# Squares folded on VectorE, a later second softmax, and expert weights loaded and split one step ahead

## The reference, cut to what matters

```python
# q, k, v: [2, 5056, 256]
qn = q / (norm(q, axis=1) + 1e-6);  kn = k / (norm(k, axis=1) + 1e-6)
s = kn.transpose(0, 2, 1) @ qn / tau            # [2, 256, 256]
a = softmax(s);  x = (v @ a).reshape(10112, 256)
# layer 1
logits = normalised(x) @ normalised(expert_emb).T / moe_tau
e = argmax(logits);  gate = softmax(logits)[e]
x = gate * (relu(x @ w1[e]) @ w2[e])
# layer 2
logits = x @ w_gate;  e = argmax(logits);  gate = softmax(logits)[e]
eom = sigmoid(x @ w_output_gate)[e]
out = gate * eom * (relu(x @ w1b[e]) @ w2b[e])
```

## Time and profile before

| | us |
|---|---|
| median of three runs | 1398.2 (1398.1 to 1405.37) |
| the profiled execution, its own time | 1400.51 |
| its span | 1398.8 |
| busy PE, DVE, ACT, POOL | 1280.1, 714.8, 497.9, 343.9 |
| share of the span on the chain that ended last: PE | 74% |
| same chain: DMA | 4% |

### The profile page before, as it was taken

One profiled execution on the slowest core, in us unless ns is written; L12 is line 12 of the kernel. 1 busy time (PEld: TensorE's weight loads), 2 busy tenths in 40 slices (PEclk: granted clock), 3 DMA queues, 4 the chain that ended last, 5 costly groups with the idle time before them and its releaser, 6 DMA issues.

```text
span 1398.8 us, 28869 instructions
## 1 busy us (share of the span) xinstructions
PE 1280.1 (92%) x10174; PEld 1249.5 (89%) x10175; DVE 714.8 (51%) x2506; ACT 497.9 (36%) x1181; POOL 343.9 (25%) x475
## 2 busy tenths in 40 slices
PE   7998853889999999999999994899999999999996
PEld 6887743879999999999999993899999999999996
DVE  5557871235555565556565562134444445444454
ACT  6448751223333233423333331233333324333333
POOL 1003773122212212221221212132222222222223
PEclk9999986999999999999999996999999999999998
DMA  8655655871111111311111115941111113111112
GB/s 314 247 196 192 216 177 187 276 263 51 46 39 39 46 33 45 99 38 33 45 41 36 46 31 189 372 128 48 45 46 46 46 42 104 42 46 46 46 50 83
DMA packets 78872, 143.88 MB, mean 103 GB/s; under 512 B 8900, under 2 KB 57679, under 8 KB 77808
## 3 DMA queue, kind: packets, MB, share of 16 engines
q1 hardware_dynamic: 54048, 92.68, 20.3%
q0 software_dynamic: 12288, 31.74, 6.1%
q10 hardware_dynamic: 12496, 18.97, 4.0%
HBM read 107.31 MB, written 38.57 MB: 104 GB/s over the span
## 4 chain that ended last, share of the span: by engine, by line
PE 74%; DMA 4%; issue 1%; SPq 1%; POOL 1%; DVE 1%; ACT 1%; DVEq 0%; POOLq 0%; ACTq 0%
PE ps L1482 32%; PE ps L1498 31%; PE ps L1391 3%; PE ps L1405 3%; PE ps L1437 2%; DMA x_in<-dispatched 2%; DMA raw<-in_moe_w_dram 2%; PE ps L1398 1%; PE ps L1428 1%; POOL dispatched L604 1%; DMA x_in_even<-dispatched 0%; SPq L374 0%; POOL w_lo L618 0%; DMA dispatched<-y_out,y_pos_i 0%; DVE w_lo L990 0%
## 5 line engine op out<-in xcount | busy, mean ns | idle before, releaser
L875 ACT ACTIVATE h_hi<-ps 128x256 fp32r<-128x256 f32 x624 | 239.6, 384 | 637.6 <-PE ps L1482 632.2
L1248 DVE SCALAR_TENSOR_TENSOR h_lo<-ps,h_hi 128x256 fp32r<-128x256 f32 x624 | 264.1, 424 | 194.7 <-ACT h_hi L875 185.7
L1498 PE MATMUL ps<-w_hi,h_hi 128*128 128x256 f32 x1248 | 362.9, 291 | 0.0
L1482 PE MATMUL ps<-xT_hi,w_hi 128*128 128x256 f32 x1248 | 360.2, 289 | 1.4 <-DVE w_lo L990 1.4
L1498 PE MATMUL ps<-w_hi,h_lo 128*128 128x256 f32 x1248 | 353.1, 283 | 0.0
L1498 PE MATMUL ps<-w_lo,h_hi 128*128 128x256 f32 x1248 | 353.1, 283 | 0.0
L1482 PE MATMUL ps<-xT_hi,w_lo 128*128 128x256 f32 x1248 | 352.8, 283 | 0.0
L1482 PE MATMUL ps<-xT_lo,w_hi 128*128 128x256 f32 x1248 | 352.7, 283 | 0.0
L1498 PEld LDWEIGHTS ps<-w_lo,h_hi 128*128 128x128 f32 x1248 | 239.0, 192 | 0.0
L1498 PEld LDWEIGHTS ps<-w_hi,h_lo 128*128 128x128 f32 x1248 | 238.8, 191 | 0.0
L1498 PEld LDWEIGHTS ps<-w_hi,h_hi 128*128 128x128 f32 x1248 | 238.7, 191 | 0.0
(11 more groups left out here) (217 smaller groups left out, 1666.7 us busy)
## 6 DMA issues: line engine op xcount, KB each, us to landing
x_in<-dispatched SPq DMA_DIRECT2D x80, 264.0 KB, 2.7
arena<-in_moe_w_dram SPq DMA_DIRECT2D x14, 1024.0 KB, 9.3
raw<-in_moe_w_dram SPq DMA_DIRECT2D x12, 1024.0 KB, 8.0
raw<-in_moe_w_dram ACTq DMA_DIRECT2D x10, 1024.0 KB, 7.4
arena<-in_q_dram SPq DMA_DIRECT2D x14, 640.0 KB, 4.9
arena<-in_k_dram SPq DMA_DIRECT2D x14, 640.0 KB, 6.3
v_sb<-in_moe_w_dram SPq DMA_DIRECT2D x8, 1024.0 KB, 7.4
v_sb<-in_v_dram SPq DMA_DIRECT2D x4, 1280.0 KB, 6.9
```

Source lines behind the costliest of these rows:

```text
L875: nc.scalar.activation(h_hi[:, c, :], h_ps(c, SUB * P), ACT.Relu).then_inc(h_hi_ready[c], 1)
L1248: V.scalar_tensor_tensor(h_lo[:, c, :], h_ps(c, SUB * P), 0.0, h_hi[:, c, :], op0=ALU.max, op1=ALU.subtract).then_inc(h_ready[c], 1)
L1482: last = T.matmul(h_ps(c, SUB * P), w1_halves[w][:, par, d, c * P:(c + 1) * P], x_halves[x][:, d, :], start=(d == 0 and at == 0), stop=(d ...
L1498: last = T.matmul(y_ps[:, s * C:(s + 1) * C], h_halves[h][:, c, s * P:(s + 1) * P], w2_halves[w][:, par, c, :], start=(c == 0 and at == 0) ...
```

## The change

Eight edits. (1) The first unit's first slot of q and of k is loaded by DMAs of its own. (2) DVE folds the five slots of `sumsq` into one by six additions, and `fold_norms` on PE shrinks from 15 products to 3. (3) The second batch's raw products are copied from PSUM to SBUF after v unit 0 (`save_s`), and `fold_norms(1)` moves from unit 0 to unit 2. (4) The rest of the second softmax moves: roots to unit 5 (beside the root of group 0), reciprocals to unit 10, scaling to 11, exponentials to 12, `make_a` to 13, the transposes and the product to units 13 to 16, and the splits to 16 and 17. The load of tail weights that waits for it moves from v group 3 to group 5. (5) SP loads only the first full expert in the prologue; ACT loads expert i + 1 before the tiles of expert i. (6) The first expert is split wholly in tail step 4 on ACT, and its w1 low half on DVE after the x of the first tile. (7) w1 and w2 of the next expert are both split behind the tiles of its predecessor, on ACT, DVE and POOL. (8) The waits for loads at a layer's end go, and two pairs of semaphores are merged.

```diff
@@ -444,6 +447,14 @@
                     sp.wait_ge(qk_squared, n - QRING + 1)
+                if n == 0:
+                    for t, src in enumerate((q[0], k[0])):
+                        rows = src[0:FULL * P, :].rearrange("(p t) c -> p t c", t=FULL)
+                        sp.dma_start(qk[:, 0, t, 0:C], rows[:, 0, :]).then_inc(qk_first, 16)
+                    for t, src in enumerate((q[0], k[0])):
+                        rows = src[0:FULL * P, :].rearrange("(p t) c -> p t c", t=FULL)
+                        sp.dma_start(qk[:, 0, t, C:].rearrange("p (t c) -> p t c", c=C), rows[:, 1:U, :]).then_inc(qk_in[0], 16)
+                    continue
                 load_unit(qk[:, n % QRING, 0, :], q[b], j, qk_in[n % QRING])
...
@@ -452,7 +463,7 @@
                     load_tail_w2(sp, 0, 0)
-                if n == 3:
+                if n == 5:
                     sp.wait_ge(a_ready, B)
...
@@ -501,14 +512,14 @@
 
-                def load_expert(r):
+                def load_first_expert():
                     sp.wait_ge(order_ready, m + 1)
...
                         sp.wait_ge(raw_free, 1)
-                    e = sp.value_load(plan[m][0:1, EXPERT, r:r + 1], min_val=0, max_val=E - 1)
-                    load_weights(sp, m, e, r)
+                    e = sp.value_load(plan[m][0:1, EXPERT, 0:1], min_val=0, max_val=E - 1)
+                    load_weights(sp, m, e, 0)
 
...
@@ -529,12 +540,11 @@
                 next_w2(5, 2)
-                load_expert(0)
+                load_first_expert()
                 next_w1(6, 3)
...
                 next_w2(7, 4)
-                load_expert(1)
 
...
@@ -655,13 +665,13 @@
 
-                def ahead(pair, par, first):
+                def behind(pair, par, first):
                     unless_last(pool, pair, par, lambda: split_w2_lo(L, pair * 2 + (par + 1), 1 - par))
...
 
-                each_tile(pool, m, nothing, body, tile, big, (ahead, None))
+                each_tile(pool, m, nothing, body, tile, big, (None, behind))
 
...
@@ -777,17 +789,17 @@
                     square_x(u - 1)
+                    if u == PAIRS:
+                        norm_roots(1)
                     if u % PAIRS == 0:
...
                     exps(u // PAIRS)
-                if u == 1:
-                    norm_roots(1)
-                if u == 4:
+                if u == 12:
                     s_exps(1)
-                if u == 8:
+                if u == 14:
                     take_aT(1)
-                if u == 10:
+                if u == 16:
                     split_a(1)
...
@@ -836,10 +845,9 @@
                             take_yT(n)
-                        if n == TP - 1:
-                            w1_piece(L, 0, 0, i)
                         if n == TP:
-                            w2_piece(L, 0, 0, i)
+                            for w in range(2):
+                                (w1_piece if i < SUB else w2_piece)(L, 0, 0, 2 * (i % SUB) + w)
                     if n < TP:
...
@@ -856,15 +864,18 @@
                     hold(act, L.w2_split_dve, 2 * pair + (par + 1))
-                    with act.If(pair < E // 2 - 1):
-                        at = nc.s_assert_le(2 * pair + (2 + par), E - 2 + par)
+
+                    def do():
+                        at = nc.s_assert_le(2 * pair + (par + 1), E - 1)
                         e = act.value_load(plan[m][0:1, EXPERT, bass.ds(at, 1)], min_val=0, max_val=E - 1)
-                        load_weights(act, m, e, par)
-                        act.reg_add(loads[par], loads[par], 1)
+                        load_weights(act, m, e, 1 - par)
+
+                    unless_last(act, pair, par, do)
 
...
                         split_w1_hi(L, pair + par, 1 - par)
+                        split_w2_hi(L, pair + par, 1 - par)
                         act.reg_add(splits, splits, 1)
...
@@ -878,13 +889,8 @@
                         y_exps(n)
-                    with act.If(t < 1):
-                        hold(act, L.tile_done, n)
-                        unless_last(act, pair, par, lambda: split_w2_hi(L, pair + par, 1 - par))
 
                 each_tile(act, m, before_expert, body, tile, big, (None, behind))
-                for r in range(2):
-                    hold(act, L.raw_in[r], act.snap(loads[r]) * 32)
                 hold(act, L.w1_split, act.snap(splits))
...
@@ -926,7 +932,11 @@
 
-            def scale_s(b):
+            def save_s(b):
+                for c in range(CC):
+                    V.tensor_copy(s_sb[:, c, :], s_ps(b, c)).then_inc(s_saved, 1)
+
+            def invert_norms(b):
                 dve.wait_ge(small_in, 80)
...
@@ -935,9 +945,12 @@
                 V.tensor_scalar(norms[:, C:], norms[:, C:], rtau[:, 0:1], None, op0=ALU.mult)
+
+            def scale_s(b):
+                dve.wait_ge(s_saved, CC * (b + 1))
                 dve.drain()
                 for c in range(CC):
-                    V.scalar_tensor_tensor(s_sb[:, c, :], s_ps(b, c), norms[:, C + c:C + c + 1], norms[:, 0:C],
+                    V.scalar_tensor_tensor(s_sb[:, c, :], s_sb[:, c, :], norms[:, C + c:C + c + 1], norms[:, 0:C],
                                                   op0=ALU.mult, op1=ALU.mult)
...
@@ -969,10 +982,20 @@
                 dve.wait_ge(square_used, b * (2 * NU - 2) + 2 * NU)
-                dve.sem_inc(sumsq_ready, 1)
+                for t in range(2):
+                    V.tensor_tensor(sumsq[:, t, 0:2 * C], sumsq[:, t, 0:2 * C], sumsq[:, t, 2 * C:4 * C], op=ALU.add).then_inc(sumsq_folded[0], 1)
+                dve.wait_ge(sumsq_folded[0], 2 * b + 2)
+                for t in range(2):
+                    V.tensor_tensor(sumsq[:, t, 0:C], sumsq[:, t, 0:C], sumsq[:, t, C:2 * C], op=ALU.add).then_inc(sumsq_folded[1], 1)
+                dve.wait_ge(sumsq_folded[1], 2 * b + 2)
+                for t in range(2):
+                    last = V.tensor_tensor(sumsq[:, t, 0:C], sumsq[:, t, 0:C], sumsq[:, t, 4 * C:], op=ALU.add)
+                last.then_inc(sumsq_ready, 1)
                 if b == 0:
...
                     V.tensor_copy(enT[:, :, :], en_ps).then_inc(enT_ready, 1)
+                    save_s(0)
+                    invert_norms(0)
                     scale_s(0)
...
@@ -1075,13 +1098,17 @@
                         split_v(ahead)
-                if u == 3:
+                if u == 1:
+                    save_s(1)
+                if u == 10:
+                    invert_norms(1)
+                if u == 11:
                     scale_s(1)
-                if u == 5:
+                if u == 13:
                     make_a(1)
-                if u == 10:
+                if u == 16:
                     take_ae(1)
-                if u == 11:
+                if u == 17:
                     split_a(1)
...
@@ -1227,16 +1254,19 @@
                         take_xT(L, n + 1)
+                        split_w1_lo(L, 0, 0)
                     if m == 0:
                         y_route_2(n)
-                    if n == TP - 1:
-                        split_w1_lo(L, 0, 0)
                     if n == TP:
...
                 def behind(pair, par, first):
-                    unless_last(dve, pair, par, lambda: split_w1_lo(L, pair * 2 + (par + 1), 1 - par))
+                    def do():
+                        split_w1_lo(L, pair * 2 + (par + 1), 1 - par)
+                        split_w2_lo(L, pair * 2 + (par + 1), 1 - par)
+
+                    unless_last(dve, pair, par, do)
                     take_y(L, dve.snap(tile))
...
@@ -1258,8 +1288,6 @@
                         y_route_2(n)
-                    with dve.If(t < 1):
-                        unless_last(dve, pair, par, lambda: split_w2_lo(L, pair * 2 + (par + 1), 1 - par))
 
...
@@ -1301,12 +1329,9 @@
                 pe.wait_ge(sumsq_ready, b + 1)
-                for t in range(U):
-                    T.matmul(norm_ps[b][0], ones[:, :], sumsq[:, 0, t * C:(t + 1) * C], start=t == 0, stop=t == U - 1)
+                T.matmul(norm_ps[b][0], ones[:, :], sumsq[:, 0, 0:C], start=True, stop=True)
                 for c in range(CC):
-                    for t in range(U):
-                        last = T.matmul(norm_ps[b][1][:, c:c + 1], sumsq[:, 1, t * C + c * P:t * C + (c + 1) * P], ones[:, 0:1],
-                                        start=t == 0, stop=t == U - 1)
+                    last = T.matmul(norm_ps[b][1][:, c:c + 1], sumsq[:, 1, c * P:(c + 1) * P], ones[:, 0:1], start=True, stop=True)
                 last.then_inc(norm_done, 1)
...
@@ -1315,8 +1340,11 @@
                         multiply_ae(0)
-                    pe.wait_ge(qk_in[j % QRING], qk_count(b, j))
                     for t in range(U):
+                        if b == 0 and j == 0 and t == 0:
+                            pe.wait_ge(qk_first, 32)
+                        elif t == (b == 0 and j == 0):
+                            pe.wait_ge(qk_in[j % QRING], qk_count(b, j))
                         r = REST if j == NU - 1 and t == U - 1 else P
...
```

(8 more changed lines are left out.)

20 lines of the change are left out of this document (11 added, 9 removed).

## The result

| | before | after |
|---|---|---|
| median | 1400.12 us (4 runs, 1398.1 to 1405.37) | 1380.47 us (4 runs, 1376.6 to 1382.84) |
| ratio | | 0.9851, 95% interval 0.9813 to 0.989 |
| the profiled execution, own time | 1400.51 | 1381.58 |
| its span | 1398.8 | 1379.8 |

The time lies in the wide range, 2.5 us inside its upper end; it is 9.5 us above the point and outside the 1364 to 1378 that the prediction gave its own sum. The profiled execution is 19 us shorter, where the sum had 27.2.

A forecast was written before the change was run, and what follows sets the result against it. PE, with 74% of the chain, bounds the kernel, so gains come only where it stands; before layer 0 the scatters bound. Terms summed to -27.2 us, 1400.5 to 1373.3, median 2.3 lower: 1371 us, 8-in-10 range 1360 to 1383.

The forecast's parts named there:

- The v stage: Ahead of layer 0: first positions 12.7 us earlier, 4.6 given back, so the stage ends 8.1 us earlier (4 to 11).
- The hole: POOL's scatters in the v stage: a gap of 4.1 us between first and second positions, before the eleventh scatter.
- The first products: Kernel start: a smaller first load lets PE do four products in advance, 0.4 us won (0.5 lost to 1.2 won).
- First fold: PE between the two batches: 6 of 30 instructions remain, 3.6 us less (3.4 to 3.8).
- Tails of layer 0 and first tile: Layer 0: waits for ACT and x go, 5.7 and 8.4 us won; the first tile's stall goes, 4.8 won.
- Changes of expert: Next expert's h_hi waits for splits: 0.3 us net won in layer 0, 3.0 lost over two changes in layer 1.
- 1.5 follows in slow products: Change of expert in layer 0: slow PE products after its stall cost 1.5 us, within 4.5 lost.
- End of layer 0: Before layer 0's last y: ACT's copy of y waits for POOL's split, 2.1 us lost (1 to 4).
- Tails of layer 1: Layer 1's tail steps: ACT's 9.92 us wait goes but DMAs are full, so 5 us won (0 to 8).
- PE waits for tail weights in step 4: Tail steps: one of the signs that would show the prediction wrong.
- changes of expert cost more: Rival, chance 0.10: POOL's pieces or ACT's hold take 2.5 us more at four places, giving 1381 us.
- The tails wait for DMA anyway: Rival, chance 0.08: weights come last in the tails, half of 19.1 us is kept, giving 1381 us.

The follow-up runs named there:

- softmax_early: The changed kernel with the second softmax back in the early units, folds on DVE and copy of raw products kept: 1379.66 us, ratio 0.9851.
- attention_part: The kernel before with edits 1 to 4 alone, expert weights loaded and split as before: 1397.56 us, ratio 0.9981.
- no_spare_split: The changed kernel without the next expert's load and splits where that expert has no full tile; engines read the tile count first: 1409.52 us, ratio 0.9817.
- dve_splits: The changed kernel with POOL's two pieces of w2's low half done by DVE at expert changes and layer ends: 1403.2 us, ratio 0.9781.
- changed_third: The changed kernel, unaltered, run again as the base in the third series: 1382.03 us, ratio 0.987 to the kernel before.
- experts_part: The kernel before with edits 5 to 8 alone, expert weights loaded and split one step ahead: 1389.77 us, ratio 0.9915.
- changed_again: The changed kernel, unaltered, run again as the base in the second series: 1381.46 us, ratio 0.9863 to the kernel before.

## Why the prediction was right, and where it was short

**The v stage** (-8.1): right in its sum in the first trace, -8.5 at the last scatter, and 1.1 and 3.5 us too much by the two others (-7.0, -4.6). The hole is where it was put and 0.5 us larger than said. What it says of causes is not all right. It booked 7.3 us as won by moving fold and softmax together, and 4.6 as given back. softmax_early shows that the softmax costs POOL's end the same at both places, so the two entries cancel but for the folds.

**The first products** (0.4 won): wrong, and outside its bounds. By the runs with the whole load the cut costs 0.9 to 2.6 us. The step that failed is "the other four slots land later by two issues": the issues are 0.95 of the 2.04 us by which they come later. Against the kernel before the fold starts 0.5 us late, against the changed kernel with the whole load 1.3. That the latter is 0.8 earlier than the kernel before, with the same load, is not explained: the same 160 products take 36.85 us in the one and 37.61 in the other.

**First fold** (-3.6): from 45.38 to the next product 0.9 us, before 4.4.

**Tails of layer 0 and first tile** (-14.1, -4.8): -14.1 and -4.7. Not foreseen was that these terms and the one of the v stage hang on each other: without them the v stage's gain was lost again in layer 0's tails, 3.9 of 4.4 us in the trace of attention_part, and the median moved by 2.2 us and not by 8.3.

**Changes of expert** (-0.3 and +3.0): the chain was right in each link, by under half a microsecond at each place: PE waits 3.48 us and not 3.0, then 1.9 and 1.7 and not 1.5. The term that was mis-sized is "1.5 follows in slow products" in layer 0 (4.8), and in layer 1, where I charged none, 1.8 each time. That makes 3.3 + 3.6 of the missing 8.2. How much it is differs from execution to execution (see the last section); that it was near its most in the profiled one is chance. Moving the guard takes waits and slow products away together.

**End of layer 0** (+2.1): +3.9. The failed step is that the last y is late through ACT's copy alone. It is late on DVE already: by DVE's own two further pieces (1.3 us), and by POOL's pieces, which hold DVE's copy of `y_id` for 2.7 us, as dve_splits shows. Leaving all splits out at this place won 5.0 us (no_spare_split), leaving out POOL's alone 0.7, as DVE took them over.

**Tails of layer 1** (-5.0): -6.0, with two waits for tail weights, 1.3 and 1.6 us, in line with the reasoning by DMA rate. The second of them is in step 4, at 884.49 us, and "PE waits for tail weights in step 4" was one of the signs of being wrong; as the term came out all the same, the sign was badly chosen for this layer.

**The rivals.** The time came out, in part by chance, at that of "changes of expert cost more" (1381, chance 0.10): 9.2 us more than forecast at those four places, where the rival had 10. Its mechanism accounts for a part: POOL and DVE hold each other up at the end of layer 0, and POOL's scatter at the change is 0.5 us long for it. The larger part is the clock, 6.9 of the 9.2 us. The Trainium skill (SBUF — State Buffer, Who interferes with whom, and SBUF: two separate sides) says that the two share a pair of ports, that a DVE instruction with two SBUF inputs contends with a GpSimd instruction that reads SBUF, and that whichever starts first holds the pair for its whole length. A subtraction of 0.7 us that lasts until POOL's two pieces are over agrees; that the profile has it start 0.35 us ahead of the first of them is not settled by any run here. The copy of `y_id` has one input, so that sentence does not reach it; that POOL's pieces held it too is what dve_splits shows. "The tails wait for DMA anyway" was wrong for both halves together, and is what happens to the first half alone.

## What to carry to other kernels

A wait that only guards a later load belongs behind the work that others wait for: moved behind one tile's `h_hi` on ACT's stream it was worth 10.6 to 14.5 us, where the whole change had won 19. Price a stall of PE by its wait and by the slow products behind it, from a row that had a wait of that length, and see whether the wait can be made short enough for the clock to stay up. And before adding up two gains, ask what the second place waits for: here 3.9 of 4.4 us won ahead of a stage were lost again within it, because its end was set by the DMAs.

## What the runs showed of the hardware

- The same wait costs differently. The 3.5 us at the change in layer 0 were followed by 4.8 us of slow products in the first trace, and by 2.3 to 4.8 in the five others that have that wait (2.3 in changed_third, 4.8 in experts_part). In the first trace the first change in layer 1 has a PE wait of 1.9 us and takes 15.6 us; in the second (changed_again) the wait is 1.9 too and the tile takes 14.1. Granted clock in the 14 us around each (columns as above):

```profile
1129.00:1143.00 14.00, 12.08 (x89) 11.87 (x88) 8.00 (x18) 6.14 (x15) 5.64 (x6) 0.88 0.47 148
```

```profile
1132.00:1146.00 14.00, 12.08 (x102) 11.87 (x101) 8.69 (x21) 7.24 (x17) 5.63 (x6) 1.00 0.43 145
```

  Waits of 0.7 and 0.5 us there (dve_splits) left the tiles at 12.9 and 12.7.
- A DVE copy of 128x2 elements from SBUF to SBUF took 2.88 us, and a subtraction of 128x512 some 3.4, beside two subtractions of POOL that last 2.5 together. Indirect DMAs issued by POOL took 1.10 to 1.50 us beside DVE's subtractions, and 0.98 and 0.99 at the same place without them (no_spare_split, end of layer 0).
- The v stage can run at a lower clock for a whole series: 0.80 to 0.84 and not 1.00 from 140 to 180 us, with groups up to 19.5 us apart and not 12.4. All four kernels profiled there had it, and the nine executions of the kernel before took 1431.0 to 1438.8 us. What set it off is open.
